# Exponentials taken from PSUM row group by row group with accumulated sums, and the second layer's weight factors prepared one eighth per tile with their rounding on ScalarE

## The reference, cut to what matters

```
def _attn_ref(q, k, v):                      # 8 batches, 8 heads, 576 rows, head size 64
    k_p = k.reshape(B, H, Sp, pool, D).mean(axis=3)      # keys pooled by 8: 72 keys
    v_p = v.reshape(B, H, Sp, pool, D).mean(axis=3)
    scores = scale * np.matmul(q, k_p.transpose(0, 1, 3, 2))
    scores = scores - np.max(scores, axis=-1, keepdims=True)
    attn = np.exp(scores)
    attn = attn / (np.sum(attn, axis=-1, keepdims=True) + 1e-09)
    return np.matmul(attn, v_p)

x = attention output as (4608, 512)
h = x @ w_in;  x = np.maximum(0.01 * h, h) @ w_out       # layer 1, d_ff = 2048
h = x @ w_in2; x = (h * clip(h + 3, 0, 6) / 6) @ w_out2  # layer 2
```

## Time and profile before

| | us |
|---|---|
| median of 3 runs | 1793.36 |
| lowest and highest | 1792.47, 1794.03 |
| the profiled execution | 1795.66 |
| its span, first to last instruction | 1793.9 |

### The profile page before, as it was taken

One profiled execution on the slowest core, in us unless ns is written; L12 is line 12 of the kernel. 1 busy time (PEld: TensorE's weight loads), 2 busy tenths in 40 slices (PEclk: granted clock), 3 DMA queues, 4 the chain that ended last, 5 costly groups with the idle time before them and its releaser, 6 DMA issues. The chain is left out here.

```text
span 1793.9 us, 34434 instructions
## 1 busy us (share of the span) xinstructions
PE 1713.4 (96%) x10794; PEld 1513.2 (84%) x10794; DVE 1032.4 (58%) x1786; ACT 623.1 (35%) x1249; POOL 696.9 (39%) x773
## 2 busy tenths in 40 slices
PE   7888889999999999999999999999999999999999
PEld 7676778888888888888889888988898989888898
DVE  8664755767767677675544555444444444444444
ACT  4443333323333233333222334333433343333333
POOL 5667867666855667522220424120303030312200
PEclk8898999999999999999999999999999999999999
DMA  5744567776867768665757775766666676757562
GB/s 142 236 128 148 186 224 241 249 247 208 272 208 253 231 213 261 214 220 172 223 177 245 213 233 175 214 198 201 202 191 219 176 216 179 219 177 215 176 200 80
DMA packets 218111, 366.81 MB, mean 204 GB/s; under 512 B 22464, under 2 KB 47040, under 8 KB 218048
## 3 DMA queue, kind: packets, MB, share of 16 engines
q1 hardware_dynamic: 218048, 366.04, 65.9%
HBM read 308.28 MB, written 57.67 MB: 204 GB/s over the span
## 5 line engine op out<-in xcount | busy, mean ns | idle before, releaser
L1341 PE MATMUL ps_h<-xs_hi,ring 128*128 128x256 f32 x3808 | 819.3, 283 | 22.6 <-issue 8.5
L1341 PEld LDWEIGHTS ps_h<-xs_hi,ring 128*128 128x128 f32 x3808 | 642.2, 189 | 72.8 <-issue 37.6
L1341 PE MATMUL ps_h<-xs_lo,ring 128*128 128x256 f32 x1904 | 533.7, 280 | 0.0
L1341 PEld LDWEIGHTS ps_h<-xs_lo,ring 128*128 128x128 f32 x1904 | 359.7, 189 | 27.8
L921 ACT ACTIVATE g_hi<-gate 128x512 fp32r<-128x512 f32 x288 | 182.0, 632 | 452.9 <-DVE gate L1101 260.8
L718 POOL TENSOR_TENSOR xs_lo<-x_stage,xs_hi 128x512 fp32r<-128x512 f32 x51 | 74.8, 1466 | 464.3 <-ACT xs_hi L893 464.3
L1134 DVE TENSOR_TENSOR u<-ps_h,p 128x256 f32<-128x256 f32 x272 | 114.5, 421 | 208.4 <-PE ps_h L1341 186.9
L1293 PE MATMUL ps_y<-g_hi,wout_hi 128*128 128x512 f32 x576 | 229.3, 398 | 0.2
L1295 PE MATMUL ps_y<-g_hi,wout_lo 128*128 128x512 f32 x576 | 228.5, 397 | 0.0
L1293 PE MATMUL ps_y<-wout_hi,g_hi 128*128 128x512 f32 x576 | 226.2, 393 | 1.4 <-DVE y_stage L1130 1.4
L1295 PE MATMUL ps_y<-wout_hi,g_lo 128*128 128x512 f32 x576 | 227.0, 394 | 0.0
(11 more groups left out here) (127 smaller groups left out, 2417.9 us busy)
## 6 DMA issues: line engine op xcount, KB each, us to landing
ring<-w_in_split SPq DMA_DIRECT2D x920, 256.0 KB, 2.8
w_in_split<-ring SPq DMA_DIRECT2D x56, 256.0 KB, 4.0
w_in_split<-stage SPq DMA_DIRECT2D x56, 256.0 KB, 3.4
k_raw<-in_kT SPq DMA_DIRECT2D x32, 288.0 KB, 3.7
q_raw<-in_qT SPq DMA_DIRECT2D x32, 288.0 KB, 4.4
v_raw<-in_v SPq DMA_DIRECT2D x32, 288.0 KB
x0T<-x_stage SPq DMA_DIRECT2D x32, 288.0 KB, 4.1
x1T<-y_stage SPq DMA_DIRECT2D x36, 256.0 KB, 3.6
```

The lines of the kernel that those rows point to most:

```text
L1341: mm = pe.matmul(banks[BANK_OF[r]], a, b[:, r, c, :], start=r in OPENS and c == 0 and n == 0, stop=c == 1 and n == 2, skip_group_check=True)
```

## The change

**Exponentials.** The subtraction on DVE goes. DVE makes a bias per row group, minus the scaled maximum (`row_bias`, two 96x6 instructions per unit). ACT takes the exponential of each 96x72 row group straight from PSUM with its own bias and lets the instruction accumulate the row sum: 6 instructions per half and 12 per unit instead of 2. The sums on DVE go. The stage `exp` becomes `exp0` and `exp1`, one place apart. `normalize` waits for the exponentials of both halves. For units 1 and 3 `normalize` and `divide` move to the third place of the step and `turn_p0` one place later.

**Factors.** Tiles 2 to 6 make one eighth each, tile 7 makes eighths 5 and 6, tile 8 makes eighth 7. The rounding moves from POOL (multiplication by one) to ACT (`factor2_hi`, a copy, one per place from place 19 on; in tile 7 from places 16 and 40, in tile 8 from place 16). POOL keeps the sums and the remainders. SP loads the raw weights at place 2 and stores from place 21; in tiles 7 and 8 it does both between the streams of the first product's factors.

```
-STAGES = ("split_qk", "scores", "exp", "normalize", "divide", "turn_p0", "pv0", "turn_p1", "pv1")
-UNIT_PLACES = [(0, 3, 4, 5, 6, 9, 11, 12, 14),
-               (11, 15, 16, 17, 18, 20, 23, 24, 26),
-               (23, 27, 28, 29, 30, 33, 35, 36, 38),
-               (35, 39, 40, 41, 42, 44, 47, 48, 50)]
+STAGES = ("split_qk", "scores", "exp0", "exp1", "normalize", "divide", "turn_p0", "pv0", "turn_p1", "pv1")
+UNIT_PLACES = [(0, 3, 4, 5, 6, 7, 9, 11, 12, 14),
+               (11, 15, 16, 17, 19, 19, 21, 23, 24, 26),
+               (23, 27, 28, 29, 30, 31, 33, 35, 36, 38),
+               (35, 39, 40, 41, 43, 43, 45, 47, 48, 50)]
...
-RAW2_PLACES = (1, 26)
-STORE2_PLACES = (19, 31)
+RAW2_PLACE = 2
+ROUND2_PLACE = 19
+STORE2_PLACE = 21
...
@@ POOL
-            def factors2(i):
+            def sums2(i):
                 pool.wait_ge(raw2_loaded, 64 * (i + 1))
                 pool.wait_ge(prep2_ready, PRODUCTS * i + 1)
                 s_sums(HF + i)
+
+            def factors2_lo(i):
                 for at, k in enumerate(PREP_ORDER):
                     slot = stage2[:, at % SLOTS2]
-                    if k in S_AT:
-                        pool.wait_ge(s_summed, 4 * (HF + i) + S_AT[k] + 1)
-                    pool.wait_ge(prep2_stored[at % SLOTS2], stored2(i, at))
                     source = s_sum[:, S_AT[k]] if k in S_AT else raw_s[:, RAW_AT[k]]
-                    nc.gpsimd.tensor_tensor(slot[:, 0:2], source, ones, ALU.mult
-                                            ).then_inc(prep2_hi_ready, 1)
                     pool.wait_ge(prep2_hi_ready, PRODUCTS * i + at + 1)
                     nc.gpsimd.tensor_tensor(slot[:, 2:4], source, slot[:, 0:2].bitcast(F32),
                                             ALU.subtract).then_inc(prep2_ready, 1)
...
@@ ACT
+            def factor2_hi(i, at, T):
+                k = PREP_ORDER[at]
+                if k in S_AT:
+                    act.wait_ge(s_summed, 4 * (HF + i) + S_AT[k] + 1)
+                else:
+                    act.wait_ge(raw2_loaded, 64 * (i + 1))
+                act.wait_ge(x_ready, PRODUCTS * T)
+                act.wait_ge(prep2_stored[at % SLOTS2], stored2(i, at))
+                nc.scalar.activation(stage2[:, at % SLOTS2, 0:2],
+                                     s_sum[:, S_AT[k]] if k in S_AT else raw_s[:, RAW_AT[k]],
+                                     ACT.Copy).then_inc(prep2_hi_ready, 1)
...
-                if name == "exp":
-                    for half in range(2):
-                        act.wait_ge(shifted, 2 * n + half + 1)
-                        nc.scalar.activation(u.prob[:, half], u.prob[:, half], ACT.Exp,
-                                             scale=SCORE_SCALE).then_inc(exp_ready, 1)
+                if name in ("exp0", "exp1"):
+                    half = int(name[-1])
+                    act.wait_ge(bias_ready, 2 * n + half + 1)
+                    above_zero(act, p_turned, 2 * freed(b, c))
+                    for r in range(HALF_SUB * 2):
+                        rows_exp = nc.scalar.activation(
+                            u.prob[:, half, r], u.ps[0:ROWS, half, r * KEYS:(r + 1) * KEYS],
+                            ACT.Exp, bias=u.row_bias[:, half, r:r + 1], scale=SCORE_SCALE,
+                            accum_out=u.row_sum[:, half, r:r + 1])
+                    rows_exp.then_inc(exp_ready, 1)
...
+                    for eighth, begins in prepares:
+                        if 0 <= HF * i + m - begins < PRODUCTS:
+                            factor2_hi(eighth, HF * i + m - begins, T)
...
@@ DVE
-                    above_zero(dve, p_turned, 2 * freed(b, c))
                     for half in range(2):
                         dve.wait_ge(max_ready, 2 * n + half + 1)
-                        nc.vector.tensor_tensor(u.prob[:, half], scores(u, half),
-                                                spread(u.row_max[:, half]), ALU.subtract
-                                                ).then_inc(shifted, 1)
+                        nc.vector.tensor_scalar(u.row_bias[:, half], u.row_max[:, half],
+                                                -SCORE_SCALE, None, ALU.mult
+                                                ).then_inc(bias_ready, 1)
                 if name == "normalize":
-                    for half in range(2):
-                        dve.wait_ge(exp_ready, 2 * n + half + 1)
-                        nc.vector.tensor_reduce(u.row_sum[:, half], u.prob[:, half], AXIS_X,
-                                                ALU.add).then_inc(sum_ready, 1)
-                    dve.wait_ge(sum_ready, 2 * n + 2)
+                    dve.wait_ge(exp_ready, 2 * n + 2)
```

More of the change, by code:

```diff
@@ L189, in ffn_attention_kernel @@
         three = sb("three", [P, 1])
-        one = sb("one", [P, 1])
         ps_y = psum("ps_y", [P, DC, 512])
@@ L215, in ffn_attention_kernel @@
         three_ready = sem("three_ready")
-        one_ready = sem("one_ready")
         v_zeroed = sem("v_zeroed")
@@ L473, in attention_at, with prep2_at, attention_tile @@
                         load_x0(T + 1, c, T + 1)
-            def prep2_at(T, place):
-                for part in range(2):
-                    i = 2 * (T - PREP_TILES[0]) + part
-                    if place == RAW2_PLACES[part]:
-                        load_raw2(i)
-                    if 0 <= place - STORE2_PLACES[part] < PRODUCTS:
-                        store_prep2(i, place - STORE2_PLACES[part])
-            def attention_tile(T, next_unit=True, prepares=False):
+            def prep2_at(i, place):
+                if place == RAW2_PLACE:
+                    load_raw2(i)
+                if 0 <= place - STORE2_PLACE < PRODUCTS:
+                    store_prep2(i, place - STORE2_PLACE)
+            def attention_tile(T, next_unit=True):
                 for i in range(HF):
@@ L564, in _ @@
             with sp.Fori(*PREP_TILES) as T:
-                attention_tile(T, prepares=True)
+                attention_tile(T)
             attention_tile(ATT_TILES - 1, next_unit=False)
-            for slot in range(SLOTS2):
-                sp.wait_ge(prep2_stored[slot], stored2(HF, slot))
             for c in range(PAIRS):
@@ L580, in _ @@
             for i in range(HF):
-                stream_step(T, i, w1_in_split, w2_in_split)
+                if i == HF - 2:
+                    for slot in range(SLOTS2):
+                        sp.wait_ge(prep2_stored[slot], stored2(HF, slot))
+                for r in range(PRODUCTS):
+                    stream(T, i, r, w1_in_split, w2_in_split)
+                    if i == 2:
+                        store_prep2(7, r)
+                if i == 0:
+                    load_raw2(7)
                 if i == 1:
@@ L740, in factors2 @@
                                             ALU.subtract).then_inc(prep2_ready, 1)
-            ones = one[:].unsqueeze(2).to_broadcast([P, 2, P])
             def stores2_done(i):
@@ L749, in _ @@
             pool.memset(three[:], 3.0).then_inc(three_ready, 1)
-            pool.memset(one[:], 1.0).then_inc(one_ready, 1)
             pool.sem_inc(prep2_ready, 1)
@@ L1003, in first_step, with step @@
                         next_x(0, i, m - 1)
-            def step(T, i, layer, before=None, attention=False, turns=True):
+            def step(T, i, layer, before=None, attention=False, turns=True, prepares=()):
                 s = HF * T + i
@@ L1059, in _ @@
                 step(1, i, 1, before=0, attention=True)
-            with act.Fori(2, ATT_TILES) as T:
+            with act.Fori(*PREP_TILES) as T:
                 for i in range(HF):
-                    step(T, i, 1, attention=True)
+                    step(T, i, 1, attention=True,
+                         prepares=[(T - PREP_TILES[0], ROUND2_PLACE)])
             for i in range(HF):
-                step(ATT_TILES, i, 1)
+                step(ATT_TILES - 1, i, 1, attention=True, prepares=[(4, ROUND2_PLACE)])
             for i in range(HF):
-                step(TILES - 1, i, 1)
+                step(ATT_TILES, i, 1, prepares=[(5, 2 * HF), (6, 5 * HF)])
+            for i in range(HF):
+                step(TILES - 1, i, 1, prepares=[(7, 2 * HF)])
                 if i == HF - 2:
```

63 lines of the change are left out of this document (36 added, 27 removed), and 4 rows, old and new, of the table FIRST_STAGES.

## The result

The changed kernel takes 1810.7 us (median of 4 runs, 1807.8 to 1813.1), the kernel before 1793.1 beside it (4 runs): a ratio of 1.0102, with a 95% interval of 1.0080 to 1.0123. So the change is slower, by 0.6 to 1.2%, or some 11 to 22 us (15 to 18 by the medians). The profiled execution has a span of 1806.0 us against 1793.9. It is the fastest of the four, so its 12.1 us are on the low side.

The account below looks back on a forecast made before the run. PE, busy for 96% of the span, was taken as the bound, so only its waits count. Preparation -12.5, softmax in tiles 1 to 6 +30.6, ahead of tile 1 +6: +24 us, 1817 us; 8 in 10 from 1783 to 1843.

Parts of the forecast that it names:

- The named signs: Trace after: tiles 2 to 5 some 2 us longer, tile 6 about 6, more PE waits for `c11` and `pT_lo`.
- The spacing, 0.36: On ACT, small exponentials follow each other every 0.36 us, without overlap or cost for the sum; a half takes 2.2 us.
- the first rival: On ACT, small exponentials overlap like large ones and the sum is free: spacing 0.24, 1781 us; chance 0.24.
- The rule that a hundredth of spacing is worth 3 us: Over all units, each 0.01 us of exponential spacing moves the total by 2.9 us, some 3 with the early units.
- Units 1 and 3, +1.85 each: At the end of a step, PE waits 0.85 us longer at part 4 for `c11` and 1.0 at `pv0`.
- Units 0 and 2, +0.7 each: Exponentials mostly fill ACT's waiting time, but DVE divides and ends `pT_lo` later: PE loses 0.7 us a unit.
- The softmax in tiles 1 to 6, +30.6: Unit costs of 2 x 1.85 and 2 x 0.7 give 5.1 us a tile, 30.6 for six tiles.
- the third rival: PE's waits at `c11` and `pv0` do not add up; a third of the softmax cost remains: 1793 us, chance 0.11.
- Ahead of tile 1, +6: Eight early units: ACT needs 3.2 us more each, DVE 1.9 less; half the difference, 0.7 each, makes +6.
- The preparation, -12.5: Five eighths in attention tiles cost 1.2 us each instead of eight at 2.45: 13.5 gained, 1 taken back.
- the bound of 7.4: Lower bound of the preparation's gain in tiles 2 to 5, nothing saved per eighth: 19.6 - 5 x 2.45 = 7.4 us.
- the wait for a stored slot: It stands ahead of ACT's other work; `g_hi` queues behind it with some 3 us of slack for PE.

Follow-up runs that it names:

- the preparation alone: Changed kernel with the old softmax and its places, keeping only the new factor preparation: 1788.0 us, ratio 0.9971 to the kernel before.
- both moved: Changed kernel, units 1 and 3: first-half exponentials behind the `c11` copy, normalize and divide behind the upper gate, tile 0 unchanged: 1798.9 us, ratio 1.0042.

## Why the prediction was right, and where it was not

The forecast was 1817 us, slower; the measured 1811 lies in the range. The named signs came too: the waits for ACT grew, tiles 2 to 5 took 1.7 us more (2 forecast), tile 6 4.7 (6 forecast), tiles 7 and 8 0.3 and 0.2. By terms:

- **The spacing, 0.36.** It is 0.295, so a half takes 1.78 us and not 2.2. The reasoning had two errors that partly cancel. Small exponentials do overlap (0.21 apart at 0.32 each), as the first rival had it from the large ones; the row of 72-column copies, which I took for the nearest, misled. And the sum does cost 0.09 of spacing, for which I took nothing. The Trainium skill, page "ScalarE: Activation LUTs", section "Rules for kernel authors", gives 0.36 by its budget. That is near the recorded length of one (0.32), but it is not the spacing of either variant, with which the prediction had it agree.
- **The rule that a hundredth of spacing is worth 3 us.** It did not hold. By it the changed kernel should have lost 20 us less than forecast, and the kernel without the accumulator 25 less again. The latter, which also has the sums back on DVE, gained 3 us in tiles 2 to 6 and nothing that the ratios could show.
- **Units 1 and 3, +1.85 each.** The mechanism, both places and nearly the size were right: 1.11 at `c11` and 1.18 at `pv0` in unit 1 of tile 6. Against the preparation alone, step 2 grew by 2.05 us and step 5 by 1.22, together 3.3 a tile of the forecast 3.7. The waits say the same: in tiles 2 to 6 that for `c11` grew from 5.0 to 13.3 us and that for `pT_lo` from 2.7 to 11.5. There is luck in the size: the exponentials were shorter than forecast, and the gate beside POOL's sums and the divisions beside its remainders were longer. The experiment with both moved shows that these handovers, and not ScalarE's load, carry the recoverable part.
- **Units 0 and 2, +0.7 each.** Over-sized. Against the preparation alone, steps 0 and 1 did not grow, and steps 3 and 4 together are 0.6 shorter, of which 0.8 is the wait for `p1` that is gone. That ScalarE's idle time covered these units is my reading; no run isolates it.
- **The softmax in tiles 1 to 6, +30.6.** It is 15.4: 13.0 in tiles 2 to 6 (555.0 - 542.0) and 2.4 in tile 1. Of the missing 15, some 8 are units 0 and 2, some 3 units 1 and 3, and 4 the wait for `p1`, which the preparation has alone and the changed kernel does not have. The longer step 2 used up that wait: the third rival's mechanism, at another place.
- **Ahead of tile 1, +6.** It is 0.7 (182.2 to 182.9). The changed kernel's repeat has 183.0 and the preparation alone 183.0 as well: the new softmax cannot be seen in this stretch. It varied from 180.2 to 186.1 us among the kernels that have the changed or the old order in tile 0, so the 180.2 of the kernel with both moves may be 2 or 3 us of luck (its granted clock there is 0.91, that of the changed kernel's repeat 0.87).
- **The preparation, -12.5.** It is -5 by the ratio and -6.6 in tiles 2 to 6. The step that failed is that half of an eighth's cost goes with half of POOL's pairs. With the preparation alone, the four eighths of tiles 2 to 5 cost 434.3 - 4 x 105.8 = 11.1 us and that of tile 6 1.9, so 2.6 each: no less than the 2.45 before (in which the lower clock of these tiles, 0.99 against 1.00, has a part too). The whole gain is that of the three eighths that went to tiles 7 and 8, the bound of 7.4 that the prediction gave for nothing saved per eighth. What the rounding took from PE's wait for `pT_lo` (6.7 to 2.7 us) it put on as a wait for `p1` (4.0). The prediction cost the wait for a stored slot at nothing, since `g_hi` queues behind it with slack; in step 3 it is `p1` that queues behind it. There it begins 3.14 us behind the start of part 0, against 1.64 before, and PE waits for 0.8 of these 1.5 us.
- **Not in the sum:** the step's 0.03 us behind tile 6, about 2 us.

So two terms that were about twice too large, one for and one against, left a total that was 6 us off by the medians, and 12 by the spans (12.1 us longer where 24 were forecast). The sign came from the right mechanism, the size partly from errors that cancelled.

The kernel with both moved is 10.8 us above the preparation alone by its median, when its profiled span is only 3.9 us longer (1794.2 against 1790.3). The other 7 us are the choice of execution: the profiled one is the fastest of six for the first (1796.0 against a median of 1798.9) and the slowest of twelve for the second (1792.1 against 1788.0).

What stays open: what the later normalization would do alone, and why the two halves together cost some 10 us less than their sum, of which the wait for `p1` explains 4.

## What to carry to other kernels

Work that is cut into small instructions on an idle engine is priced by what stands behind it in the queue at each handover, not by the engine's busy share. Move the cut work behind the handover, move its consumer behind the next one in the same edit, and look whether another phase reads the same table of places. When a second engine is relieved, look which short instructions the remaining work now falls beside. When work moves to another engine with a wait ahead of it, look at every handover that can come to stand behind that wait, and not only at the nearest. And cut a tile into steps at the engine that limits it: a border taken at another engine's late instruction puts time into the wrong step.

## What the runs showed of the hardware

- An exponential of 96x72 with a bias and an accumulated sum is followed by a separate read instruction. The groups of the changed kernel over the whole span, and under the last dots that of the kernel without the sum (its busy time is only 78.2 us, since overlapping time counts once):

```profile
L980 ACT ACTIVATE prob<-ps_att,row_bias 96x72 f32<-96x72 f32 x348 | 105.1, 323 | 52.1 <-DVE row_bias L1212 52.1
...
L980 ACT ACTIVATION_READ_ACCUMULATOR prob<-ps_att,row_bias 96x1 f32 x348 | 73.4, 211 | 0.0
...
L981 ACT ACTIVATE prob<-ps_att,row_bias 96x72 f32<-96x72 f32 x348 | 78.2, 324 | 54.2 <-DVE row_bias L1212 54.2
```

  The read is recorded at 211 ns but adds only 0.09 us to the spacing (0.295 against 0.21).
- Instructions of DVE with two operands in SBUF took longer beside POOL: the gate (128x512) 0.69 us alone and 1.09 to 1.21 beside POOL's sums, two divisions (96x432) 1.12 and 2.15 beside its remainders.
- The length of a step bound by matmuls depends on the SBUF address of buffers that are moved by a few dozen bytes: 10.47 us unmoved, 10.50 at 48 bytes, 10.56 at 64. What in the address decides, and which of the moved buffers, was not tried further.
